# Attention outputs written from PSUM into the operand of the gated MLP, weight rows loaded in the matching order, and one attention phase in every MLP step

## The chip, the cores and the metric

The kernel runs on one core of one Trainium2 chip. The metric is the device time of one execution in microseconds, as the median of several runs. Everything is float32 at the boundary. The large matrix products take their operands as two float32r parts, high and low.

## What is computed

```python
# attention: B, H, S, D = 4, 8, 768, 48
for t in range(S):
    cur = einsum('bhd,bhe->bhde', u * k[t], v[t])
    y[t] = einsum('bhd,bhde->bhe', r[t], state + cur)
    state = w[t][..., None] * state + einsum('bhd,bhe->bhde', k[t], v[t])
x = y.transpose(0, 2, 1, 3).reshape(3072, 384)      # channel = 48 * head + d
x = ((x @ w_a) * (x @ w_b)) @ w_out                 # 384 -> 1536 -> 384
h = x @ w_in                                        # 384 -> 2048
out = (maximum(h, 0) + alpha * minimum(h, 0)) @ w_out2
```

## The kernel before, in words

**Attention** (in `front`). The sequence recurrence is replaced by a tree. Inside blocks of 64 positions the weights of query and key pairs are built in a leaf step and in levels of 2 to 64, by multiplying decays into keys and queries; between blocks a state per head is carried. The work is cut into 8 duos. A duo is half the sequence (384 tokens) of four pairs of heads of one batch. It has two streams, j = 0 and 1, of two pairs each (a pair of one stream is a unit); the two heads of a pair lie in partitions 0 to 47 and 64 to 111. A duo has 11 phases: leaf products (phase 0), the products of w on DVE (phase 1, no TensorE work), five levels of 192 small products (2 to 6; levels 1 to 4 on blocks of 64, level 5 on 32), the turning of keys (7), key-value products of stream 0 and of stream 1 (8, 9), and outputs (10): `weighted_values` of both streams, then `state_products`, accumulated in banks 0 to 3 of the PSUM tensor `products`, with the heads of stream 1 crossed (partition 64 * (hd ^ j)).

**From attention to the MLP.** ACT copies the outputs to `f_y` (`copy_y`, L478), SP stores them to `y` in DRAM by four DMAs per duo (`store_y`, L306), then loads a tile of 384 tokens and all 384 channels into `x_in` (`load_tile`, L333; `load_x`, L114), ACT makes `x_hi` (L122) and DVE `x_lo` (L126). `f_y` also holds the products of w of a duo, so `products_of_w` (L754) waits until the stores have landed.

**The gated MLP** runs on 8 tiles of 384 tokens in 12 steps each (f, 128 hidden channels): `up_a` and `up_b` of 9 products of 128x384 each (3 channel blocks by 3 products hi*hi, lo*hi, hi*lo; L132), ACT's copy of a, DVE's product `g_sb` (L862), ACT's `g_hi`, DVE's `g_lo` (L868) and `down`, again 9 products. The tile's result goes to `x_in` (`copy_x2`, L507) and to DRAM for the second MLP, called leaky, which follows in a block of its own and is not touched but for the counts that it waits for.

**Order.** Every engine runs a list written out by hand. The first BEFORE_TILES = 13 phase steps run alone; then `step_at(g)` (L167) puts one phase into each of the steps f = 0 to 10 of every tile, none into f = 11. In a step with a phase the order on TensorE is up_a(g), down(g - 1), up_b(g), phase; the b product then shares bank 4 with a (`shared_bank`, L179, and `b_ps`, L271) and has to wait for ACT's copy of a. Elsewhere it goes to bank 0 or 1.

**Weights.** A piece is 128x768 numbers (256 columns of w_a or w_b, or 256 rows of w_out). SP loads it into one of three `stage` buffers with one DMA (L97), ACT makes the high part (L103), POOL the low part (L108). Piece n is loaded once piece n - 3 is split. The first EARLY = 5 pieces are split in the opening, in steps 6, 7, 8, 9 and 11; `new_pieces(f)` (L189) names those of tile 0's steps. The queue of SP is in order: per duo it issues v and r (phase 2), k (7), the stores of y, the loads of w (10), and between them pieces and x.

## Time and profile before

| | us |
|---|---|
| median of 3 runs | 1073.93 (1073.47 to 1075.55) |
| the profiled execution, its own time | 1074.55 |
| its span, first to last instruction | 1072.7 |
| TensorE (PE) busy | 1011.1, 94% |
| DVE busy | 502.3, 47% |
| ACT busy | 302.5, 28% |
| POOL busy | 218.8, 20% |
| mean granted TensorE clock | 0.98 |

PE is the row of TensorE's products, PEld that of its weight loads, SPq and ACTq the queues that issue DMAs. A row of a group gives the busy time, the mean time of one in ns, then the idle time of the engine just before them and what ended it. A row of the timeline gives start and length in us; what stands in brackets is the idle time before it and what ended it. The granted clock is a share of 2.4 GHz.

### The profile page before, as it was taken

How to read it: one execution, taken by the hardware profiler on the slowest of the kernel's cores; microseconds unless marked ns; L12 is line 12 of the kernel's file. 1: busy time of each engine (PE TensorE's matmuls, PEld its weight loads, DVE VectorE, ACT ScalarE, POOL GpSimd, SP SyncE). 2: the span in 40 equal slices, each digit the busy share in tenths (PEclk: the TensorE clock that was granted, in tenths of full speed). 3: DMA queues.
4: the chain of work that ended last, by engine and by line, in shares of the span. 5: the costliest groups of instructions: out<-in, count | busy, mean ns of one | idle time of the engine just before them, and what ended most of it. 6: DMA issues, size and time to landing. Idle time of an engine off the chain costs nothing. (4 is left out here: it accounts for less than half of the span.)

```text
span 1072.7 us, 28894 instructions
## 1 busy us (share of the span) xinstructions
PE 1011.1 (94%) x12448; PEld 982.5 (92%) x12448; DVE 502.3 (47%) x978; ACT 302.5 (28%) x612; POOL 218.8 (20%) x165
## 2 busy tenths in 40 slices
PE   4658899999999999999999998999999999999998
PEld 4548899899899999899999998999999999999998
DVE  6367344344353453443353223645454545454554
ACT  2423422422323323224213332421212121222221
POOL 3456424024043132131140140400000000000000
PEclk9769999999999999999999999999999999999999
DMA  6342450140231221311300221310101010101000
GB/s 175 101 135 76 116 156 3 45 125 6 65 101 28 72 72 28 92 51 28 94 24 3 73 98 60 96 45 1 45 2 45 1 44 0 44 0 46 1 23 23
DMA packets 45687, 60.09 MB, mean 56 GB/s; under 512 B 4096, under 2 KB 45568, under 8 KB 45568
## 3 DMA queue, kind: packets, MB, share of 16 engines
q1 hardware_dynamic: 44240, 58.21, 18.3%
q8 instruction: 94, 1.54, 0.6%
q10 hardware_dynamic: 1328, 0.13, 0.1%
q14 instruction: 25, 0.20, 0.1%
HBM read 44.17 MB, written 14.16 MB: 54 GB/s over the span
## 5 line engine op out<-in xcount | busy, mean ns | idle before, releaser
L134 PE MATMUL products<-x_hi,weights_hi 128*128 128x384 f32 x576 | 202.9, 352 | 22.7 <-DVE x_lo L128 21.0
L135 PE MATMUL products<-x_lo,weights_hi 128*128 128x384 f32 x576 | 195.8, 340 | 0.0
L136 PE MATMUL products<-x_hi,weights_lo 128*128 128x384 f32 x576 | 195.6, 340 | 0.0
L862 DVE TENSOR_TENSOR g_sb<-a_g,products 128x384 f32<-128x384 f32 x96 | 53.2, 554 | 275.6 <-PE products L136 188.9
L995 DVE TENSOR_SCALAR leaky_low<-leaky_h_ps,leaky_al 128x384 f32<-128x384 f32 x128 | 79.0, 617 | 176.5 <-PE leaky_h_ps L136 176.4
L947 ACT ACTIVATE leaky_g_hi<-leaky_g_sb 128x384 fp32r<-128x384 f32 x128 | 67.3, 525 | 295.7 <-DVE leaky_g_sb L1000 295.7
L134 PEld LDWEIGHTS products<-x_hi,weights_hi 128*128 128x128 f32 x576 | 109.2, 190 | 28.9 <-DVE x_lo L128 23.1
L388 POOL TENSOR_TENSOR r_in<-r_in,f_y 112x384 f32<-112x384 f32 x80 | 104.9, 1325 | 143.9 <-PE products L602 143.9
L434 ACT ACTIVATE g_hi<-g_sb 128x384 fp32r<-128x384 f32 x96 | 50.4, 525 | 250.4 <-DVE g_sb L862 250.4
L136 PEld LDWEIGHTS products<-x_hi,weights_lo 128*128 128x128 f32 x576 | 109.5, 190 | 0.0
L135 PEld LDWEIGHTS products<-x_lo,weights_hi 128*128 128x128 f32 x576 | 109.4, 190 | 0.0
L134 PE MATMUL acc<-g_hi,weights_hi 128*128 128x384 f32 x288 | 98.6, 343 | 3.6 <-DVE g_lo L868 3.6
L136 PE MATMUL acc<-g_hi,weights_lo 128*128 128x384 f32 x288 | 98.1, 341 | 0.0
L135 PE MATMUL acc<-g_lo,weights_hi 128*128 128x384 f32 x288 | 97.6, 339 | 0.0
L434 ACT ACTIVATE a_g<-products 128x384 f32<-128x384 f32 x96 | 47.1, 491 | 135.4 <-PE products L136 135.3
L868 DVE TENSOR_TENSOR g_lo<-g_sb,g_hi 128x384 fp32r<-128x384 f32 x96 | 61.7, 643 | 40.7 <-ACT g_hi L434 40.6
L977 DVE TENSOR_TENSOR leaky_g_lo<-leaky_g_sb,leaky_g_hi 128x384 fp32r<-128x384 f32 x128 | 74.7, 584 | 5.3 <-ACT leaky_g_hi L947 4.7
L602 PEld LDWEIGHTS products<-r_in,k_in 48*64 48x64 f32 (+1 forms) x3840 | 61.5, 139 | 16.4 <-issue 11.4
L602 PE MATMUL products<-r_in,k_in 48*64 48x32 f32 (+1 forms) x3840 | 66.4, 223 | 6.5 <-DVE a_sb L784 3.8
L1000 DVE SCALAR_TENSOR_TENSOR leaky_g_sb<-leaky_h_ps,leaky_low 128x384 f32<-128x384 f32 x128 | 70.5, 551 | 0.3
L134 PE MATMUL leaky_h_ps<-x_hi,ahead_hi 128*128 128x384 f32 x192 | 65.4, 341 | 2.4 <-PEq L197 2.4
L134 PE MATMUL leaky_acc<-ahead_hi,leaky_g_hi 128*128 128x384 f32 x192 | 64.6, 337 | 0.7 <-DVE leaky_g_lo L977 0.7
(72 smaller groups left out, 1844.3 us busy)
## 6 DMA issues: line engine op xcount, KB each, us to landing
x_in<-y_dram SPq DMA_DIRECT2D x16, 576.0 KB, 4.6
k_in<-in_k_dram SPq DMA_DIRECT2D x16, 336.0 KB, 4.2
r_in<-in_r_dram SPq DMA_DIRECT2D x16, 336.0 KB, 5.2
w_v<-in_w_dram SPq DMA_DIRECT2D x16, 336.0 KB, 5.0
stage<-in_w_out_dram SPq DMA_DIRECT2D x14, 384.0 KB, 3.1
w_v<-in_v_dram SPq DMA_DIRECT2D x16, 288.0 KB, 3.1
y_dram<-f_y SPq DMA_DIRECT2D x32, 144.0 KB, 2.7
y_dram<-x_in SPq DMA_DIRECT2D x8, 576.0 KB, 3.3
```

Source lines behind the costliest of these rows:

```text
L134: pe.matmul(out, w_hi, x_hi, start=first, stop=False)
L135: pe.matmul(out, w_hi, x_lo, start=False, stop=False)
L136: return pe.matmul(out, w_lo, x_hi, start=False, stop=last)
L388: pool.tensor_tensor(halves(t, h, 1), halves(t, h, 1), decay(j, h, 0), ALU.mult).then_inc(r_stepped[j], 1)
L434: return act.activation(out, in_, ACT.Copy)
L602: last = pe.matmul(view(products, level_bank(phase, hd) + 32 * (CH * j + c), [[1, 32]], rows, BLOCK * par), key_blocks(k_in[j], hd, c, par ...
L862: dve.tensor_tensor(g_sb[:, :], a_g[:, :], b_ps(g), ALU.mult).then_inc(g_ready, 1)
L868: dve.tensor_tensor(g_lo[f % 2][:, :], g_sb[:, :], g_hi[f % 2][:, :].bitcast(F32), ALU.subtract).then_inc(g_lo_ready, 1)
L947: return act.activation(out_, in_, ACT.Copy)
L977: return dve.tensor_tensor(out_, in_, hi.bitcast(F32), ALU.subtract)
L995: dve.tensor_scalar(low[f % 2][:, :], h, 0.0, al[:, f:f + 1], ALU.min, ALU.mult).then_inc(low_ready, 1)
L1000: dve.scalar_tensor_tensor(g_sb[f % 2][:, :], h, 0.0, low[f % 2][:, :], ALU.max, ALU.add).then_inc(g_ready, 1)
```

## The change

- `copy_outputs` (ACT) and `lower_outputs` (DVE) read the output banks of `products` and write the high and the low part of x: stream 0's two units and stream 1's first unit (rows 0 to 111) go to the three channel blocks of `x_parts`, which is `x_hi` and `x_lo` in one tensor. Stream 1's second unit goes to the second half of `f_y`, and six DMAs of 16 rows move it to rows 48 to 63 and 112 to 127 of the three blocks (`move_rows`; for duo 0 two of them on ACT's queue). The DRAM trip of y, `store_y`, `load_tile` and the x splits of the first MLP go, except those of x for the second MLP's first tile.
- The channels of x now lie in another order, so the rows of w_a and w_b are loaded in that order: six DMAs per piece (`heads_in_place`) of 48 rows x 2 KB, 48 rows x 1 KB and 16 rows x 3 KB, twice. The number of bytes is the same.
- BEFORE_TILES is 11, and every step from g = 0 has a phase until all are done (g = 76). Step 0 counts as a shared-bank step. EARLY is 3: three pieces are split in the opening, their high parts in phases 2 to 4, their low parts in phases 7 to 9; the others in tile 0.
- `weighted_values` of stream 0 runs in phase 9, after the key-value products of stream 1.
- In the opening, DVE merges stream 0's leaf before it steps stream 1's keys, and stream 1's leaf before the five smaller products of w of stream 1. For duo 0 the preparation of duo 1's keys and of its second stream's queries stands behind the outputs.

```diff
 PIECE = 2 * P * KT
-EARLY = 5
+EARLY = 3
 AHEAD = 8
...
 F_AT = {2: 0, 4: S // 2, 8: S // 2 + S // 4, 16: S - S // 8, 32: S - S // 16, 64: S - S // 32}
-BEFORE_TILES = PHASES + 2
-EARLY_AT = [6, 7, 8, 9, 11]
-X_SPLIT = 10
+BEFORE_TILES = PHASES
+LO_AT = [7, 8, 9]
+HI_AT = [2, 3, 4]
+X_LOAD, X_SPLIT = 4, 8
+OUTPUTS, MOVES = 6, 6
 STAGES = 3
...
         self.x_in = sb("x_in", [P, KT * TT])
-        self.x_hi = [sb(f"x_hi{j}", [P, KT * TT], F32R) for j in range(2)]
-        self.x_lo = [sb(f"x_lo{j}", [P, KT * TT], F32R) for j in range(2)]
+        self.x_parts = [sb(f"x_parts{j}", [P, 2 * KT * TT], F32R) for j in range(2)]
+        self.x_hi, self.x_lo = ([x[:, part * KT * TT:(part + 1) * KT * TT] for x in self.x_parts] for part in range(2))
         self.staged, self.x_loaded = [sem(f"staged{j}") for j in range(STAGES)], sem("x_loaded")
...
-        self.pieces, self.number, self.place = [], {}, {}
+        self.pieces, self.number, self.place, self.staged_by = [], {}, {}, {}
         for ups, down in up_down:
...
                 for name, w in ups:
-                    self._add(name, n, w[:, 2 * P * n:2 * P * (n + 1)].rearrange("(k p) n -> p k n", p=P), [[2 * P, KT], [1, 2 * P]])
-                self._add("down of " + ups[0][0], n, down[2 * P * n:2 * P * (n + 1), :].rearrange("(f p) m -> p f m", p=P), [[DM, 2], [1, DM]])
-
-    def _add(self, name, n, source, dims):
-        self.number[name, n] = len(self.pieces)
-        self.pieces.append((source, dims))
+                    columns = w[:, 2 * P * n:2 * P * (n + 1)]
+                    if len(ups) > 1:
+                        self._add(name, n, self.heads_in_place(columns))
+                    else:
+                        self._add(name, n, [(0, P, 0, [[2 * P, KT], [1, 2 * P]], columns.rearrange("(k p) n -> p k n", p=P))])
+                self._add("down of " + ups[0][0], n, [(0, P, 0, [[DM, 2], [1, DM]],
+                                                       down[2 * P * n:2 * P * (n + 1), :].rearrange("(f p) m -> p f m", p=P))])
+    def heads_in_place(self, columns):
+        dims = [[1, 2 * P]]
+        parts = []
+        for block in range(2):
+            row0, last = 64 * block, D * (7 - block)
+            parts.append((row0, D, 0, [[2 * P, 2]] + dims, columns[0:2 * E2, :].rearrange("(k r) n -> r k n", k=2)[D * block:D * (block + 1)]))
+            parts.append((row0, D, 4 * P, dims, columns[D * (5 - block):D * (6 - block), :]))
+            parts.append((row0 + D, 16, 0, [[2 * P, KT]] + dims, columns[last:last + D, :].rearrange("(k p) n -> p k n", p=16)))
+        return parts
+    def _add(self, name, n, parts):
+        at = self.number[name, n] = len(self.pieces)
+        self.pieces.append(parts)
+        self.staged_by[at] = self.staged_by.get(at - STAGES, 0) + 16 * len(parts)
...
     def load_piece(self, sp, n):
-        source, dims = self.pieces[n]
         if n >= STAGES:
             sp.wait_ge(self.w_ready, n - STAGES + 1)
-        sp.dma_start(view(self.stage[n % STAGES], 0, dims, P), source).then_inc(self.staged[n % STAGES], 16)
+        for row0, rows, at, dims, source in self.pieces[n]:
+            sp.dma_start(view(self.stage[n % STAGES], at, dims, rows, row0), source).then_inc(self.staged[n % STAGES], 16)
...
         (hi, _), at = self.place[n]
-        act.wait_ge(self.staged[n % STAGES], 16 * (n // STAGES + 1))
+        act.wait_ge(self.staged[n % STAGES], self.staged_by[n])
         act.activation(hi[:, at:at + PIECE], self.stage[n % STAGES][:, :], ACT.Copy).then_inc(self.w_hi_ready, 1)
...
-    tile, f = divmod(g, F1)
-    step = BEFORE_TILES + PHASES * tile + f
-    return step if f < PHASES and step < DUOS * PHASES else None
+    step = BEFORE_TILES + g
+    return step if step < DUOS * PHASES else None
...
-    return slot_at(g - 1) and slot_at(g)
+    return g == 0 or (slot_at(g - 1) and slot_at(g))
...
                 return BANK * (2 * j + side)
+            def output_parts(n):
+                hi, lo = shared.x_hi[n % 2], shared.x_lo[n % 2]
+                last_hi, last_lo = f_y[:, S:S + TT].bitcast(F32R), f_y[:, S + TT:2 * S].bitcast(F32R)
+                units_of_0 = (0, 2, hi[0:ROWS, 0:2 * TT], lo[0:ROWS, 0:2 * TT])
+                units_of_1 = ((1, 1, last_hi, last_lo), (0, 1, hi[0:ROWS, 2 * TT:3 * TT], lo[0:ROWS, 2 * TT:3 * TT]))
+                parts = []
+                for j, par, group in ((1, 0, units_of_1), (1, 1, units_of_1), (0, 0, (units_of_0,)), (0, 1, (units_of_0,))):
+                    for unit, units, hi_ap, lo_ap in group:
+                        ps = view(products, stream_bank(j, par) + TT // 2 * unit, [[BLOCK, HALF * units], [1, BLOCK]])
+                        tokens = [ap.rearrange("p (c t) -> p c t", t=P)[:, :, BLOCK * par:BLOCK * (par + 1)] for ap in (hi_ap, lo_ap)]
+                        parts.append((j, ps, *tokens))
+                return parts
+            def move_rows(engine, n, q, row0):
+                to = shared.x_parts[n % 2][row0 + D:row0 + 64, :].rearrange("p (h c) -> p h c", h=2)[:, :, q * TT:(q + 1) * TT].bitcast(F32)
+                engine.dma_start(to, f_y[row0 + 16 * q:row0 + 16 * q + 16, S:2 * S].rearrange("p (h t) -> p h t", h=2)).then_inc(moved, 16)
...
-                def store_y(n, j):
-                    first = 4 * (n // 2) + 2 * j
-                    sp.wait_ge(copied, copies(n, "outputs", j, 1))
-                    for hd in range(2):
-                        sp.dma_start(y[first:first + 2, hd, :, TT * (n % 2):TT * (n % 2 + 1)].rearrange("u d s -> d u s"),
-                                     view(f_y, S * j, [[TT, 2], [1, TT]], D, 64 * (hd ^ j))).then_inc(y_stored[j], 16)
+                def move_last_unit(n):
+                    sp.wait_ge(copied, outputs_copied(n, OUTPUTS - 1))
+                    sp.wait_ge(lowered, outputs_lowered(n, OUTPUTS - 1))
+                    for q in range(KT if n > 0 else 2):
+                        for row0 in (0, 64):
+                            move_rows(sp, n, q, row0)
...
                     elif phase == 10:
-                        store_y(n, 0)
-                        store_y(n, 1)
-                        if n == 0:
-                            load_tile(0)
+                        move_last_unit(n)
                         if n + 1 < DUOS:
...
                             load_w(n + 1, 1)
-
-                def load_tile(tile):
-                    b, half = divmod(tile, 2)
-                    if tile > 0:
-                        sp.wait_ge(shared.x_ready, tile)
-                    if tile > 1:
-                        sp.wait_ge(shared.x2_stored, 16 * (tile - 1))
-                    if tile < TILES:
-                        for j in range(2):
-                            sp.wait_ge(y_stored[j], 32 * (tile + 1))
-                    shared.load_x(sp, b % B, half)
...
                         shared.store_x2(sp, *divmod(tile - 1, 2))
-                    if f == X_SPLIT - 2:
-                        load_tile(tile + 1)
+                    if tile == TILES - 1 and f == X_LOAD:
+                        sp.wait_ge(shared.x2_stored, 16 * tile)
+                        shared.load_x(sp, 0, 0)
                 sp.wait_ge(x2_copied, TILES)
                 shared.store_x2(sp, B - 1, 1)
-                for j in range(2):
-                    sp.wait_ge(y_stored[j], 32 * DUOS)
+                sp.wait_ge(moved, 16 * MOVES * DUOS)
...
-                def copy_y(n, j):
-                    act.wait_ge(products_done[j], after(n, 9))
-                    for par in range(2):
-                        copy(view(f_y, S * j + BLOCK * par, [[P, CH], [1, BLOCK]]),
-                             view(products, stream_bank(j, par), [[BLOCK, CH], [1, BLOCK]])).then_inc(copied, 1)
+                def copy_outputs(n):
+                    if n >= 2:
+                        act.wait_ge(b_done, F1 * (n - 1))
+                    for j, ps, hi, _ in output_parts(n):
+                        act.wait_ge(products_done[j], after(n, 9))
+                        copy(hi, ps).then_inc(copied, 1)
...
                     elif phase == 10:
-                        copy_y(n, 0)
-                        copy_y(n, 1)
+                        copy_outputs(n)
+                        if n == 0:
+                            act.wait_ge(lowered, OUTPUTS)
+                            for row0 in (0, 64):
+                                move_rows(act, n, 2, row0)
...
                         prepare_r(n + 1, 0)
-                    elif phase == 8 and n + 1 < DUOS:
+                    elif phase == (10 if n == 0 else 8) and n + 1 < DUOS:
                         prepare_k(n + 1, 0)
                         prepare_r(n + 1, 1)
-                    elif phase == 9 and n + 1 < DUOS:
+                    if phase == (10 if n == 0 else 9) and n + 1 < DUOS:
                         prepare_k(n + 1, 1)
...
                     act.wait_ge(down_done, F1 * (tile + 1))
-                    act.wait_ge(shared.x_ready, tile + 2)
+                    act.wait_ge(shared.x2_stored, 16 * tile)
+                    if tile == TILES - 1:
+                        act.wait_ge(shared.x_ready, 1)
                     for m in range(KT):
...
                     attend_late(step)
-                    if step in EARLY_AT:
-                        shared.split_hi(act, EARLY_AT.index(step))
-                    if step == PHASES:
-                        shared.split_x_hi(act, 0, 0)
+                    if step in HI_AT:
+                        shared.split_hi(act, HI_AT.index(step))
                 for g in range(TILES * F1):
...
                     for j in range(2):
-                        weighted_values(n, j)
-                    for j in range(2):
                         pe.wait_ge(r_stepped[j], 6 * n + 6)
...
                         turn_keys(n, 1)
-                    elif 8 <= phase <= 9:
-                        key_values(n, phase - 8)
+                    elif phase == 8:
+                        key_values(n, 0)
+                    elif phase == 9:
+                        key_values(n, 1)
+                        weighted_values(n, 0)
                     elif phase == 10:
+                        weighted_values(n, 1)
                         outputs(n)
...
                     if f == 0:
-                        pe.wait_ge(shared.x_ready, tile + 1)
+                        pe.wait_ge(copied, outputs_copied(tile, OUTPUTS - 1))
+                        pe.wait_ge(lowered, outputs_lowered(tile, OUTPUTS - 1))
+                        pe.wait_ge(moved, 16 * MOVES * (tile + 1))
                     if tile == 0 and f % 2 == 0:
...
                         pe.wait_ge(g_ready, from0(g - 1))
-                    if f >= 10 and tile < 6:
-                        pe.wait_ge(merged, merges(tile + 2, 0, f - 10))
-                    elif f == 9 and tile == 6:
-                        pe.wait_ge(copied, copies(DUOS - 1, "outputs", 0, 1))
+                    if step_at(g) is None:
+                        pe.wait_ge(copied, outputs_copied(DUOS - 1, OUTPUTS - 1))
+                        pe.wait_ge(lowered, outputs_lowered(DUOS - 1, OUTPUTS - 1))
+                    elif not shared_bank(g):
+                        pe.wait_ge(merged, merges(step_at(g) // PHASES, 0, g % 2))
                     up(g, "w_b", b_ps(g), b_done)
...
             def _(dve):
-                def products_of_w(n, first, streams):
+                def products_of_w(n, first, streams, parts=(True, True)):
...
                     for j in range(first, first + streams):
-                        dve.wait_ge(y_stored[j], 32 * n)
+                        dve.wait_ge(moved, 16 * MOVES * n)
                         dve.wait_ge(w_loaded[j], 16 * (n + 1))
-                    dve.tensor_tensor(of(f_y, 0, 1, S // 2), of(w_v, 0, 2, S // 2), of(w_v, 1, 2, S // 2), ALU.mult).then_inc(f_done, 1)
+                    if parts[0]:
+                        dve.tensor_tensor(of(f_y, 0, 1, S // 2), of(w_v, 0, 2, S // 2), of(w_v, 1, 2, S // 2), ALU.mult).then_inc(f_done, 1)
+                    if not parts[1]:
+                        return
                     for i, h in enumerate((4, 8, 16, 32, 64)):
...
+                def lower_outputs(n):
+                    if n >= 2:
+                        dve.wait_ge(b_done, F1 * (n - 1))
+                    for part, (j, ps, hi, lo) in enumerate(output_parts(n)):
+                        dve.wait_ge(copied, outputs_copied(n, part | 1 if part < 4 else part))
+                        dve.tensor_tensor(lo, ps, hi.bitcast(F32), ALU.subtract).then_inc(lowered, 1)
                 def attend_early(step):
...
                     n, phase = divmod(step, PHASES)
-                    if phase == 0:
+                    if phase == 0 and n > 0:
                         for j in range(2):
...
                         carry_states(n, phase - 8)
+                    elif phase == 10:
+                        lower_outputs(n)
...
                 dve.memset(products[:, :], 0.0).then_inc(products_cleared, 1)
-                for j in range(2):
-                    first_step_k(0, j)
-                    products_of_w(0, j, 1)
+                first_step_k(0, 0)
+                products_of_w(0, 0, 1)
                 dve.wait_ge(leaf_mask_loaded, 32)
                 dve.wait_ge(cleared, 1)
+                merge_leaf(0, 0)
+                first_step_k(0, 1)
+                products_of_w(0, 1, 1, (True, False))
+                merge_leaf(0, 1)
+                products_of_w(0, 1, 1, (False, True))
                 for step in range(BEFORE_TILES):
-                    if step == BEFORE_TILES - 1:
-                        shared.split_x_lo(dve, 0, 0)
                     attend_early(step)
```

## Rows read from the trace of the kernel before

**Rows 1.** The page: busy TensorE, and the costliest group of DVE in the MLP.

```profile
PE 1011.1 (94%) x12448; PEld 982.5 (92%) x12448; DVE 502.3 (47%) x978; ACT 302.5 (28%) x612; POOL 218.8 (20%) x165
...
L862 DVE TENSOR_TENSOR g_sb<-a_g,products 128x384 f32<-128x384 f32 x96 | 53.2, 554 | 275.6 <-PE products L136 188.9
```

**Rows 2.** Waits of TensorE, whole span: for what, us in total, times, longest.

```profile
PE products L134 <- DVE x_lo L128: 21.0, 7, 14.3
...
PE products L657 <- issue: 5.3, 4, 1.7
...
PE acc L134 <- DVE g_lo L868: 3.6, 4, 1.5
```

**Rows 3.** Timeline from the first outputs to the first MLP product.

```profile
42.14 2.59 PE L657 MATMUL products<-r_in,state 48*48 48x64 f32 x80
...
47.65 1.59 ACT L434 ACTIVATE f_y<-products 112x384 f32<-112x384 f32 x4
...
48.55 2.84 PE L579 MATMUL products<-r_leaf,k_scratch 48*64 48x64 f32 x96 [3.82 <-ACT f_y L434]
...
50.07 2.54 SPq L310 DMA_DIRECT2D y_dram<-f_y  x4
...
61.08 4.55 DVE L128 TENSOR_TENSOR x_lo<-x_in,x_hi 128x1152 fp32r<-128x1152 f32 x1 [8.58 <-ACT x_hi L124]
...
65.69 0.69 PE L134 MATMUL products<-x_hi,weights_hi 128*128 128x384 f32 x1 [14.30 <-DVE x_lo L128]
```

**Rows 4.** Windows: us, busy us and count of each engine, granted clock, DMA share, GB/s.

```profile
40.30:65.60 25.30, 6.75 (x224) 6.38 (x224) 6.99 (x9) 8.40 (x17) 8.20 (x6) 0.50 0.43 129
65.70:71.00 5.30, 5.30 (x17) 5.30 (x18) 4.84 (x6) 1.96 (x3) 3.45 (x2) 0.50 0.09 24
```

**Rows 5.** Timeline of the opening, around the first merges of the leaf.

```profile
10.98 0.56 DVE L823 TENSOR_TENSOR k_in<-k_in,w_v 112x384 f32<-112x384 f32 x1 [0.89 <-DMA w_v<-in_w_dram]
...
13.03 1.32 DVE L766 TENSOR_TENSOR f_y<-f_y 112x192 f32<-112x192 f32 x5
...
14.28 1.98 DVE L784 COPY_PREDICATED a_sb<-leaf_mask,products 128x384 f32<-128x384 int32 x4
...
16.31 2.79 PE L602 MATMUL products<-r_in,k_in 48*64 48x32 f32 x96 [3.84 <-DVE a_sb L784]
```

**Rows 6.** Timeline of a duo in the middle, from its last output products.

```profile
287.42 0.64 PE L657 MATMUL products<-r_in,state 48*48 48x64 f32 x26 [1.19 <-issue]
...
291.36 1.44 SPq L282 DMA_DIRECT2D w_v<-in_w_dram  x2
...
296.05 1.19 POOL L394 TENSOR_TENSOR k_in<-k_in,w_v 112x384 f32<-112x384 f32 x1 [31.98 <-DMA w_v<-in_w_dram]
...
301.20 0.95 DVE L762 TENSOR_TENSOR f_y<-w_v 112x768 f32<-112x768 f32 x1
...
302.19 1.71 DVE L766 TENSOR_TENSOR f_y<-f_y 112x384 f32<-112x384 f32 x5
```

**Rows 7.** The stores of y: issue time in ns, and time to landing.

```profile
L310 SPq DMA_DIRECT2D y_dram<-f_y x32: 327/440/1052, 50.1 to 590.5; - x32
...
DMA to landing us min/median/max: 2.2/2.7/4.0
```

**Rows 8.** Timeline of POOL in the first step of tile 0.

```profile
72.55 2.87 POOL L388 TENSOR_TENSOR r_in<-r_in,f_y 112x384 f32<-112x384 f32 x2 [3.39 <-PE products L602]
75.37 3.95 POOL L111 TENSOR_TENSOR weights_lo<-stage,weights_hi 128x768 fp32r<-128x768 f32 x2
```

**Rows 9.** Groups by line: ACT's high parts of the first MLP's weights.

```profile
L106 ACT ACTIVATE weights_hi<-stage 128x768 fp32r<-128x768 f32 x18 | 14.9, 838 | 1.3 <-DMA stage<-in_w_a_dram 1.2
```

**Rows 10.** Timeline of TensorE: duo 1's last output products.

```profile
133.11 0.33 PE L657 MATMUL products<-r_in,state 48*48 48x64 f32 x8 [1.71 <-issue]
```

**Rows 11.** DMA queues from 130 to 134 us: packets, MB, share of 16 engines.

```profile
q8 instruction: 1, 0.02, 1.4%
```

**Rows 12.** Window of one duo's period, from duo 2's outputs to duo 3's.

```profile
288.00:362.60 74.60, 73.36 (x1270) 70.01 (x1268) 32.42 (x73) 23.63 (x52) 20.12 (x16) 1.00 0.21 62
```

42 lines of the change are left out of this document (23 added, 19 removed).

## The prediction

> **What bounds the kernel now.** I read the page first. TensorE is busy 1011.1 us, 94% of the span [rows 1]. So a change pays where it fills TensorE's idle time, and nowhere else. The waits of TensorE say what that time is: 21.0 us for the DVE that makes x_lo (7 times, the longest 14.3), 5.3 us of "issue" ahead of the output products of line 657, 3.6 us for g_lo [rows 2]. The other waits lie in the opening attention phases. Next I read the opening in order of time [rows 3]. The first duo's output products end at 44.7. ACT copies them to f_y only at 47.65 (it is preparing the next duo's keys), the leaf of duo 1 runs at 48.55, the stores to DRAM are issued from 50.07, x_in is loaded behind them, x_lo takes 4.55 us from 61.08 beside a busy POOL, and the first MLP product starts at 65.69. From 40.3 to 71.0 the granted clock is 0.5, the lower level, 1.2 GHz [rows 4]. TensorE had just become mostly idle before it fell, and it rose 5.3 us after dense work began again.
>
> **The change, part by part.** Times are on the span of the profiled execution. T is the end of a duo's output products.
>
> 1. *First leaf merges moved.* DVE now merges stream 0 in the idle 0.89 us it has before the second stream's w, and leaves the five small f_y products (1.32 us) behind the second merge [rows 5]. The merges were four in 1.98 us; two go ahead (0.99, of which about 0.1 sticks out), and 1.32 moves behind. TensorE's level 1 starts at about 14.2, not 16.3, and everything up to the outputs moves by 2.1 us. DVE has 1.3 us to spare during level 1, so the postponed products cost nothing. Outputs end at 44.7 - 2.1 = 42.6. Moving ACT's weight splits to phases 2 to 4, where it idles, adds nothing.
>
> 2. *Outputs straight to x, first tile.* For duo 0 the key preparations now stand behind the copies, so ACT starts at 42.7. Four copies of 384 columns took 1.59 us [rows 3]; six copies, four of half width, I take at 2.3 (between 1.6 and 2.6). DVE subtracts behind them; the last, like the product of a step at 0.55 us [rows 1], ends at 45.6. Then rows move by DMA: four issues on SP, two on ACT. The nearest row is the store of f_y: issue 0.33 to 1.05 us, median 0.44; landing 2.2 to 4.0 us, median 2.7 [rows 7]. The last of four issues starts 1.6 to 2.4 us after the first (I take 2.0), and I take 2.7 for the landing: 50.4. The first up product starts there instead of at 65.69: -15.3. Two things come back. The leaf of duo 1, done in the old idle time, now runs inside the MLP at full clock: 2.84 us at half clock [rows 3] gives about +1.6. And step 0 now uses the shared bank, so the b product waits for ACT's copy of a: +0.8 (a copy of about 0.4 and two handovers; 0.5 to 1.2). The half-clock tail of 5.3 us stays. Part sum **-12.9** (-14.5 to -9).
>
> 3. *x for later tiles.* Besides the 14.3 there are six x_lo waits of 21.0 - 14.3 = 6.7 us at tile starts [rows 2]. They go with x_lo itself: **-6.7**. Late next is the move. Duo 1's outputs end at step 10 and tile 1 starts at step 12, with 27 MLP products and the leaf between. One duo's period is 74.6 us for 12 steps and 11 phases [rows 12], 6.2 us per step, and 6.4 with this leaf. The path is copies and subtraction 3.0, six issues 2.6 to 3.3, landing 2.7: T + 8.7 against T + 6.4. **+2.3** (0 to +5). For duo 2 the slack is one step more, then two, and so on: nothing. A stall can also drop the clock for a short stretch, as after the opening [rows 4]: I add **+1.0** (0 to +3).
>
> 4. *Weight rows loaded to fit.* A w_a or w_b piece is now six DMAs instead of one. This is the part whose price I know least. It matters in tile 0, where five pairs of such pieces are split (EARLY goes from 5 to 3) and four of them loaded. A piece three ahead is loaded only when POOL has split the old one. The loop of a pair is: POOL's two splits, 3.95 us [rows 8]; twelve issues at 0.44, 5.3; the last landing, 2.7; ACT's split of 0.84 [rows 9]. Sum 12.8 us, while two steps give 12.4. POOL also has its 2.87 us of query steps per phase ahead of the splits [rows 8], but two steps hold both. So the loop is just on the path: 0.4 us in each of four pairs, plus some collisions of ACT's waiting split with g_hi. **+2.5**. Below, tile 0's g_lo waits of 3.6 us vanish; above, issues at 1.05 give rival A. One rule speaks against this part. The Trainium skill, "DMA: Bandwidth & Descriptors", "Rules for kernel authors", wants many small transfers made into one, since below 64 KB one pays mostly overhead; half of the parts and all the moved rows are of 48 KB. The stores here, 144 KB each, lie closer to one whole piece than to such a part, so no row contradicts it. If by that rule every part cost as much as the slowest store's issue, the time would be rival A's.
>
> 5. *A phase per step, no step left out.* The moves stand in SP's queue ahead of the loads of w. Today w is issued 3.3 us after T and POOL starts 4.7 us after that issue [rows 6]. Now the issue comes at T + 3.0 + 3.0 = T + 6.0 to 6.7, POOL starts at T + 11.4, and its four operations of 1.2 us end at T + 16.1. Level 1 was two full steps and an empty one behind the leaf; now it comes at T + 16.3. It just fits. DVE's products of w (0.95 and 1.71 us alone [rows 6], up to twice that beside POOL) now sit directly ahead of the step whose g_lo TensorE needs at T + 19.8; I get T + 19.4 to 20.0. **+1.5** over six duos (0 to +12).
>
> 6. *Weighted values of stream 0 in phase 9.* In the output burst the wait of 1.71 us comes in the middle of line 657's products, while one packet moves on the instruction queue [rows 10, 11]: the burst of 190 products with their weight loads outruns the fetching of code. 48 of them (0.7 us) leave the burst for a phase that had half a load. 5.3 us of such waits [rows 2] become perhaps half: **-2.6** (-5.3 to 0).
>
> 7. *Rest.* ACT and DVE lose eight x splits and gain copies of similar length. DRAM traffic falls, on no path. The second MLP is untouched.
>
> Sum: -12.9 - 6.7 + 2.3 + 1.0 + 2.5 + 1.5 - 2.6 = **-14.9 us**. The profiled execution took 1074.55 us around its span of 1072.7, and gives 1059.65; the median of the runs is 0.6 lower, so 1059.0.
>
> **The rivals.** *A, slower: SP becomes the bound.* Place: the six-part weight loads of tile 0 and the six moves ahead of each w. If an issue costs 0.9 to 1.05 us, which the slowest stores show [rows 7], not 0.44, the loop of a pair grows by 12 x 0.5 = 6 us, four times: +24. Level 1 of six duos also waits some 2 us. Time 1080 or more. It decides from about 0.7 us per issue on, where the gain is gone. Against it: the median is 0.44 and the traffic is light. Chance 0.08. *B, the DRAM trip was only part of the wait.* If the rows land as late as the slowest stores and x is ready near 54, if ACT's and DVE's queues hold the copies, and the crowding of part 5 costs 1 us a duo, the saving shrinks to some 7 us: 1067. Chance 0.18, and 0.02 more that nothing is left of it (1072 to 1076). *C, all stalls go.* Code fetching never lags and tile 0 flows freely: 1051. Chance 0.12. *Forecast*: 1059, chance 0.60.
>
> **The numbers.** About 0.2% is what a measurement of this kernel can tell from no change, 2 us. Rival A is slower; the 0.02 counts as the same; the rest, 0.90, is faster. The range 1051 to 1071 takes in the forecast with its bounds, B and most of C; it leaves out A and the lower tail.
>
> **What would show it.** Right: first up product near 50 with no load from y before it; x_lo gone from TensorE's waits; one wait of 2 to 3 us at the start of tile 1 for a DMA; "issue" ahead of line 657's successor halved; few waits for w pieces in tile 0. Wrong: SP's issues of weight parts end to end through tile 0 with ACT waiting on stage; TensorE waiting for r_in or k_in at every level 1; a start of the MLP later than 54.

## The result, and the profile after

The changed kernel takes 1067.47 us, the median of 5 runs (1065.47 to 1069.02), against 1074.19 us for the kernel before in the same comparison: ratio 0.9932 with an interval of 0.9914 to 0.9949. That is 6.7 us faster. The forecast was 14.9 us faster. The time lies inside the range of the prediction, but less than half of the saving that it forecast came.

The profiled execution took 1068.26 us, with a span of 1066.5. TensorE's row of the page answers to [rows 1]:

```profile
PE 1013.6 (95%) x12448; PEld 984.7 (92%) x12448; DVE 521.1 (49%) x1018; ACT 293.7 (28%) x620; POOL 217.7 (20%) x165
```

**Where the time went.** The first up product starts at 52.86 instead of 65.69 [rows 3], 12.8 us earlier. From there to the end the kernel before needed 1007.0 us and this one 1013.6. So 6.6 us are given back inside the MLP tiles. The prediction had 15.3 and +0.4 for these two stretches: it was 2.5 short in the first, 6.2 in the second. Two windows from just behind the first product, first of the kernel before, then of the one after, split the second. The columns are the window, its length, and the busy time of PE, PEld, DVE, ACT and POOL, then the granted clock, the DMA share and GB/s.

```profile
66.00:1072.00 1006.00, 981.18 (x11408) 954.74 (x11407) 469.25 (x915) 281.73 (x568) 190.82 (x139) 0.99 0.17 51
```

```profile
53.00:1066.00 1013.00, 985.56 (x11504) 958.79 (x11504) 493.20 (x954) 275.18 (x577) 196.16 (x143) 0.99 0.16 45
```

TensorE is busy 4.4 us longer (the 96 products of duo 1's leaf are among it now) and idle 27.4 us instead of 24.8. The idle time hardly moves although x_lo's waits are gone, so new waits took their place. TensorE's waits in the kernel after (waited for, us in total, times, longest) name them; these answer to [rows 2]:

```profile
PE acc L153 <- DVE g_lo L927: 13.1, 8, 3.8
PE products L618 <- ACT r_leaf L473: 10.6, 2, 7.7
PE products L153 <- issue: 10.5, 2, 7.6
PE acc L153 <- ACT x_in L468: 2.6, 1, 2.6
...
PE products L641 <- POOL r_in L422: 1.1, 1, 1.1
...
PE products L153 <- ACT a_g L468: 0.6, 1, 0.6
```

x_lo is gone, and the 5.3 us of "issue" in the output burst too. "issue" ahead of L153 is the wait for the moved rows: 7.63 us in the opening and 2.85 at tile 1. New are 13.1 us for g_lo, against 3.6 before, and 2.6 and 1.1 us for ACT and POOL. Looked up one by one in the timeline, they fall into two sets. Three lie in tile 0: 3.82 us up to 91.73, 0.88 and 1.85. Six lie some 20 us behind the outputs of a duo, at five places for duos 2 to 6: 2.65, 1.11 with 1.49 behind it, 1.48, 1.78 and 1.54, together 10.05 us. Each set had one experiment or more.

The second set, in the duo that answers to [rows 6]: SP's queue, DVE, POOL and TensorE of the kernel after, from the timeline (start, length; in brackets the idle time before).

```profile
285.06 3.77 SPq L316 DMA_DIRECT2D x_parts<-f_y  x6
288.88 2.32 SPq L329 DMA_DIRECT2D w_v<-in_w_dram  x2
...
294.15 1.21 POOL L428 TENSOR_TENSOR k_in<-k_in,w_v 112x384 f32<-112x384 f32 x1 [34.52 <-DMA w_v<-in_w_dram]
295.31 1.52 POOL L422 TENSOR_TENSOR r_in<-r_in,w_v 112x384 f32<-112x384 f32 x1
296.78 1.91 POOL L428 TENSOR_TENSOR k_in<-k_in,w_v 112x384 f32<-112x384 f32 x1
298.65 1.47 POOL L422 TENSOR_TENSOR r_in<-r_in,w_v 112x384 f32<-112x384 f32 x1
...
295.69 1.95 DVE L807 TENSOR_TENSOR f_y<-w_v 112x768 f32<-112x768 f32 x1
297.68 4.91 DVE L813 TENSOR_TENSOR f_y<-f_y 112x384 f32<-112x384 f32 x5
302.58 0.56 DVE L921 TENSOR_TENSOR g_sb<-a_g,products 128x384 f32<-128x384 f32 x1
...
300.18 0.90 PE L641 MATMUL products<-r_in,k_in 48*64 48x32 f32 x48 [1.11 <-POOL r_in L422]
304.34 0.44 PE L153 MATMUL acc<-g_hi,weights_hi 128*128 128x384 f32 x1 [1.49 <-DVE g_lo L927]
```

The duo's outputs end at 282.1. The six moves wait for the copies and take 3.77 us of the queue, and w is issued at T + 6.8, just past the upper end that the prediction gave (T is the end of a duo's output products, here 282.1). POOL starts 5.3 us later, T + 12.0 here, and then its four operations lie over all six of DVE's products of w. These take 1.95 and 4.91 us instead of 0.95 and 1.71 [rows 6]. g_sb stands behind them on DVE, so it, g_hi and g_lo come late, and TensorE waits.

### The profile page after: what moved, and what is told of

Its sections match the earlier page's. It is cut to its first block and busy times, and to the rows that moved or that the text cites. A ratio compares the mean times of both kernels' runs of the same rounds, so it can differ in the third digit from the quotient of the medians.

```text
span 1066.5 us, 29038 instructions
## 1 busy us (share of the span) xinstructions
PE 1013.6 (95%) x12448; PEld 984.7 (92%) x12448; DVE 521.1 (49%) x1018; ACT 293.7 (28%) x620; POOL 217.7 (20%) x165
## 3 DMA queue, kind: packets, MB, share of 16 engines
q8 instruction: 94, 1.54, 0.6%
## 5 line engine op out<-in xcount | busy, mean ns | idle before, releaser
L153 PE MATMUL products<-x_parts,weights_hi 128*128 128x384 f32 x576 | 204.0, 354 | 11.9 <-issue 10.5
L154 PE MATMUL products<-x_parts,weights_hi 128*128 128x384 f32 x576 | 196.9, 342 | 0.0
L155 PE MATMUL products<-x_parts,weights_lo 128*128 128x384 f32 x576 | 196.4, 341 | 0.0
L153 PEld LDWEIGHTS products<-x_parts,weights_hi 128*128 128x128 f32 x576 | 110.3, 192 | 16.7 <-issue 12.3
L422 POOL TENSOR_TENSOR r_in<-r_in,f_y 112x384 f32<-112x384 f32 x80 | 99.8, 1261 | 112.1 <-PE products L641 109.3
L153 PE MATMUL acc<-g_hi,weights_hi 128*128 128x384 f32 x288 | 99.6, 346 | 15.7 <-DVE g_lo L927 13.1
L154 PEld LDWEIGHTS products<-x_parts,weights_hi 128*128 128x128 f32 x576 | 110.4, 192 | 0.0
L155 PEld LDWEIGHTS products<-x_parts,weights_lo 128*128 128x128 f32 x576 | 110.4, 192 | 0.0
L927 DVE TENSOR_TENSOR g_lo<-g_sb,g_hi 128x384 fp32r<-128x384 f32 x96 | 67.3, 701 | 43.1 <-ACT g_hi L468 42.5
L153 PEld LDWEIGHTS acc<-g_hi,weights_hi 128*128 128x128 f32 x288 | 55.0, 191 | 18.7 <-DVE g_lo L927 18.6
L153 PE MATMUL leaky_h_ps<-x_parts,ahead_hi 128*128 128x384 f32 x192 | 64.7, 337 | 2.4 <-PEq L225 2.4
```

The lines of the kernel that those rows point to most:

```text
L153: pe.matmul(out, w_hi, x_hi, start=first, stop=False)
L154: pe.matmul(out, w_hi, x_lo, start=False, stop=False)
L155: return pe.matmul(out, w_lo, x_hi, start=False, stop=last)
L422: pool.tensor_tensor(halves(t, h, 1), halves(t, h, 1), decay(j, h, 0), ALU.mult).then_inc(r_stepped[j], 1)
L927: dve.tensor_tensor(g_lo[f % 2][:, :], g_sb[:, :], g_hi[f % 2][:, :].bitcast(F32), ALU.subtract).then_inc(g_lo_ready, 1)
```

## The experiments

Each edit is against the changed kernel unless another is named. Each ratio is to the kernel before, measured beside it; differences of ratios are turned into time with 1074 us. By the intervals of the two ratios such a difference is good to some 3 us either way.

**1. w ahead of the moves.** Only the order in SP's queue changes.

```diff
                     elif phase == 10:
-                        move_last_unit(n)
                         if n + 1 < DUOS:
                             load_w(n + 1, 0)
                             load_w(n + 1, 1)
+                        move_last_unit(n)
```

> The changed kernel with the loads of the next duo's w issued ahead of the six moves of rows. Theory X (w comes late behind the moves, so POOL's first steps of keys and queries collide with DVE's products of w, and DVE is late with g_sb of the phase-2 step): POOL starts about 6 us after a duo's outputs, not 9; DVE's products of w take 0.95 + 1.7 us again, not 1.95 + 4 to 5; the phase-2 waits of TensorE of 1.1 to 2.7 us (10 us over five duos, and one clock dip of 1.5) vanish; tile 1's wait for the moves grows by about 1.1 us. Time 1057 to 1060 us. Rival Y (the products of w directly ahead of a step with a phase are too much for DVE, whenever w comes): the waits stay at 1 us or more per duo, time 1066 to 1069 us.

Measured: 1052.35 us (1047.87 to 1053.06), ratio 0.9800 (0.9783 to 0.9817). These two lines are worth 14.2 us by the ratios (0.9932 less 0.9800), more than the 8 to 10 us that were expected. The same duo in its timeline:

```profile
270.50 0.81 SPq L329 DMA_DIRECT2D w_v<-in_w_dram  x2
...
273.43 3.79 SPq L316 DMA_DIRECT2D x_parts<-f_y  x6
...
274.58 1.18 POOL L428 TENSOR_TENSOR k_in<-k_in,w_v 112x384 f32<-112x384 f32 x1 [26.45 <-DMA w_v<-in_w_dram]
...
283.62 0.95 DVE L807 TENSOR_TENSOR f_y<-w_v 112x768 f32<-112x768 f32 x1
284.61 1.70 DVE L813 TENSOR_TENSOR f_y<-f_y 112x384 f32<-112x384 f32 x5
```

w is issued the moment the outputs end, POOL is through by 279.6, and DVE's products of w stand alone at 0.95 and 1.70 us. Of TensorE's waits between 145 and 636 us one is left:

```profile
PE acc L153 <- DVE g_lo L927: 0.3, 1, 0.3
```

The moves still begin where they did, behind the copies: w's two issues fit into the time in which ACT and DVE copy. Tile 1 waited 2.66 us for its rows, not more than 2.85. So the order in the changed kernel bought nothing that this run shows.

**2. Half of the moves ahead of w.**

```diff
-                    for q in range(KT if n > 0 else 2):
-                        for row0 in (0, 64):
-                            move_rows(sp, n, q, row0)
+                    rows = [(q, row0) for q in range(KT if n > 0 else 2) for row0 in (0, 64)]
+                    for at, (q, row0) in enumerate(rows):
+                        if at == len(rows) // 2 and n + 1 < DUOS:
+                            load_w(n + 1, 0)
+                            load_w(n + 1, 1)
+                        move_rows(sp, n, q, row0)
...
                         move_last_unit(n)
-                        if n + 1 < DUOS:
-                            load_w(n + 1, 0)
-                            load_w(n + 1, 1)
```

> The changed kernel with the loads of w issued behind three of the six moves. A smaller dose of the same cause. Theory X (what counts is whether POOL's four steps are done before DVE's products of w start, 13.1 us after the outputs): w is issued at +4.9 and lands at +8.9, POOL runs from +9 to +13.6, DVE's products take about 3 us, TensorE's phase-2 waits stay under 0.5 us; tile 1 waits about 4 us for the last moves, 1.1 more than in the change. Time 1053 to 1056 us. Rival (every place behind a move costs its share, 2 us of time per move): half of the 14 us come back, 1059 to 1061 us.

Measured: 1054.95 us, ratio 0.9834 (0.9814 to 0.9853). The waits behind the outputs are gone here too, with w three issues (1.8 us) earlier than after. So the cost is not so much per move: it sets in somewhere between three and six moves ahead of w. The same duo shows why. POOL ends at 290.25, 0.3 us before DVE's products of w start:

```profile
289.06 1.19 POOL L422 TENSOR_TENSOR r_in<-r_in,w_v 112x384 f32<-112x384 f32 x1
290.59 0.95 DVE L807 TENSOR_TENSOR f_y<-w_v 112x768 f32<-112x768 f32 x1
```

What w takes from the later moves now shows: tile 1 waits 4.56 us and the opening 10.03.

**3. Weight pieces whole.** w_a and w_b are loaded by one DMA per piece again; the placing of the weight rows is left out.

```diff
-                    if len(ups) > 1:
+                    if len(ups) > 9:
                         self._add(name, n, self.heads_in_place(columns))
```

> The changed kernel with w_a and w_b pieces loaded by one DMA each, in plain row order, so the rows do not match x: this leaves out the placing of weight rows, all else is as in the change. Theory P (the six-part loads cost the opening about 2 us, because the second stream's w lands 2 us later, and make tile 0's waits for g_lo of 6.6 us and two clock dips of 1.5): the first up product starts near 50.5, not 52.9, and tile 0 loses at most 3 us in waits. Time 1059 to 1061 us. Rival (tile 0's waits are POOL's splits locking out DVE, as before, whatever the loads): only the opening's 2 us come back, 1065 to 1066 us.

Measured: 1061.79 us, ratio 0.9883 (0.9860 to 0.9905), 5.3 us less than the changed kernel, with 3.1 us either way. The first up product starts at 51.0; with six parts it starts between 49.9 and 52.9 in the runs that leave the moves alone, so the opening gives nothing that shows. Tile 0, from its first up product to tile 1's, takes 85.3 us instead of 91.1. Together with experiment 1:

> The loads of w first, and w_a and w_b pieces by one DMA each in plain row order (leaves out the placing of weight rows). Theory P (six parts per piece cost tile 0 about 5 us: ACT's high part waits for the last part, holds up g_hi and pushes g_lo into POOL's splits): the wait of 3.8 us at the end of step 4 goes, tile 0 and its clock dips give back 4 to 6 us, 1047 to 1048.5 us. Rival (what was won with whole pieces before was luck of the DMAs in the opening): 1051 to 1053 us, and the waits for g_lo in tile 0 stay at 6 us.

Measured: 1045.08 us, ratio 0.9731 (0.9715 to 0.9746). The two gains add: 14.2 and 5.3 make 19.5, and 21.6 came, again more than was expected. But what do the six parts cost: issue time, or the moment at which the last of them lands?

**4. ACT's high parts behind g_hi.** In tile 0 ACT waits for a piece before it makes g_hi of the step. Here it makes g_hi first. w is ahead of the moves as in experiment 1, the parts stay six.

```diff
+                    act.wait_ge(g_ready, g + 1)
+                    act.wait_ge(down_done, from0(g - 1))
+                    copy(g_hi[f % 2][:, :], g_sb[:, :]).then_inc(g_hi_ready, 1)
                     if tile == 0:
                         for piece in new_pieces(f):
                             shared.split_hi(act, piece)
-                    act.wait_ge(g_ready, g + 1)
-                    act.wait_ge(down_done, from0(g - 1))
-                    copy(g_hi[f % 2][:, :], g_sb[:, :]).then_inc(g_hi_ready, 1)
```

> The loads of w first, and in tile 0 ACT makes the high parts of weights behind g_hi, not ahead of it. Theory H (the long g_lo wait is g_hi standing behind a split that waits for its last part): the waits for g_lo in tile 0 fall from 6.4 us to under 3, time 1047.5 to 1050 us. Rival L (the loop of load, high part, low part then turns too slowly): TensorE waits for weight pieces (lines of the first products of even steps, for POOL or DMA) by more than what g_lo gives back, 1052 us or more.

Measured: 1044.28 us (1040.65 to 1045.64), ratio 0.9715 (0.9694 to 0.9735). That is 9.1 us less than experiment 1, where 2.3 to 4.8 were expected, and at least as much as whole pieces gave there (7.4; the intervals overlap). The timeline shows why. First the kernel after, in the middle of tile 0: ACT, DVE, POOL, TensorE.

```profile
85.80 0.85 ACT L125 ACTIVATE weights_hi<-stage 128x768 fp32r<-128x768 f32 x1 [2.98 <-DMA stage<-in_w_b_dram]
86.55 0.51 ACT L468 ACTIVATE g_hi<-g_sb 128x384 fp32r<-128x384 f32 x1
...
84.70 0.56 DVE L921 TENSOR_TENSOR g_sb<-a_g,products 128x384 f32<-128x384 f32 x1 [1.71 <-issue]
...
87.10 4.58 DVE L927 TENSOR_TENSOR g_lo<-g_sb,g_hi 128x384 fp32r<-128x384 f32 x1 [0.94 <-ACT g_hi L468]
...
85.64 2.10 POOL L422 TENSOR_TENSOR r_in<-r_in,f_y 112x384 f32<-112x384 f32 x2 [1.44 <-PE products L641]
87.70 3.56 POOL L130 TENSOR_TENSOR weights_lo<-stage,weights_hi 128x768 fp32r<-128x768 f32 x2
...
91.73 0.60 PE L153 MATMUL acc<-g_hi,weights_hi 128*128 128x384 f32 x1 [3.82 <-DVE g_lo L927]
```

And the same place with g_hi first:

```profile
84.01 0.52 ACT L468 ACTIVATE g_hi<-g_sb 128x384 fp32r<-128x384 f32 x1 [3.31 <-DVE g_sb L921]
84.44 1.57 ACT L125 ACTIVATE weights_hi<-stage 128x768 fp32r<-128x768 f32 x2
...
84.80 0.55 DVE L927 TENSOR_TENSOR g_lo<-g_sb,g_hi 128x384 fp32r<-128x384 f32 x1
...
85.76 5.19 DVE L825 TENSOR_TENSOR k_in<-k_in,f_y 112x384 f32<-112x384 f32 x1
...
86.91 3.62 POOL L130 TENSOR_TENSOR weights_lo<-stage,weights_hi 128x768 fp32r<-128x768 f32 x2
```

In the kernel after g_sb is done at 85.26, but ACT stands for 2.98 us at the last part of w_b and comes to g_hi at 86.55. g_lo then starts 0.6 us before the end of a query step of POOL, behind which its two low parts follow at once, and takes 4.58 us instead of 0.55. With g_hi first, g_lo is done before POOL starts. The long operation is now a step of the keys, 5.19 us, and TensorE waits only 0.47 us for it. Tile 0 takes 82.8 us and waits 0.7 for g_lo.

**5. The same edit without experiment 1's.**

> The changed kernel with ACT's high parts behind g_hi in tile 0, and nothing else. Theory: this cost sits in tile 0 alone and the late w in the later tiles alone, so they add: 8 us off 1067.5, 1058 to 1061 us; tile 0's waits for g_lo under 1.5 us, the phase-2 waits of 1.1 to 2.7 us all still there. Rival (they share time, the one hides the other): less than 5 us off.

Measured: 1058.25 us, ratio 0.9868 (0.9840 to 0.9897): 6.9 us less than the changed kernel, tile 0 at 82.1 us, the waits behind the outputs still there (2.65, 2.01, 1.78, 1.49, 1.86). The two faults are separate.

**6. g_hi first, w first and whole pieces** (the placing of the weight rows is left out).

> The loads of w first, the high parts behind g_hi, and whole pieces in plain row order (leaves out the placing of weight rows). Theory (the six parts cost time only because ACT waits for the last part ahead of g_hi): once that wait is behind g_hi the parts are nearly free, within 1.5 us of the 1044.3 with six parts. Rival (the parts cost SP and POOL time of their own): another 4 us or more come off, 1040 us or less.

Measured: 1043.72 us, ratio 0.9727 (0.9699 to 0.9755), against 0.9715 with six parts. Once ACT no longer stands in front of g_hi, six parts cost nothing that these runs can tell (whole pieces came out 1.3 us slower, with 3.7 either way). The Trainium skill, "DMA: Bandwidth & Descriptors", "Rules for kernel authors", would have small transfers made into one; here the measurement shows no gain from it once TensorE's next step does not stand behind the last part. ACT still waits 3.4 us for parts in experiment 4 and 1.6 us for whole pieces here, and it costs no time that shows.

**7. Weighted values back in phase 10.**

```diff
                         key_values(n, 1)
+                    elif phase == 10:
                         weighted_values(n, 0)
-                    elif phase == 10:
                         weighted_values(n, 1)
```

> The changed kernel with the weighted values of stream 0 back in phase 10. Theory F (the output burst outruns the fetching of code): waits marked issue of 1 to 1.7 us return inside the output products in three or four duos, +4 to +6 us less what they hide of other waits: 1070 to 1073 us. Rival (the waits went for another reason, such as the new alignment or the DRAM traffic that is gone): no such waits, within 1 us of 1067.5.

Measured: 1069.51 us (10 runs), ratio 0.9957 (0.9941 to 0.9972), 2.7 us more than the changed kernel, with 2.5 either way; 4 to 6 were expected. In TensorE's waits "issue" returns twice in the output products, 1.8 us in all, and once, 0.7 us, in front of an up product:

```profile
PE products L696 <- issue: 1.8, 2, 1.1
```

The place is the one that was named, but only two duos have such a wait, where three or four were expected, and only 1.8 of the 5.3 us of the kernel before come back. So the move explains a third of what vanished. Why the rest is gone is not shown.

**8. The first pieces of weights loaded later.** In the profiled execution after, w of the second stream landed just ahead of 12.97 us, when DVE takes it up, where the kernel before had 10.98 [rows 5]. The suspicion was the traffic of three pieces that are now loaded in eighteen parts.

```diff
-                for piece in range(STAGES):
-                    shared.load_piece(sp, piece)
                 for step in range(BEFORE_TILES):
                     attend(step)
+                    if step == 2:
+                        for piece in range(STAGES):
+                            shared.load_piece(sp, piece)
```

> The changed kernel with the first three weight pieces (13 DMAs) issued after the values and the next queries, not ahead of them. Theory P: the second stream's w lands near 11.0 us, not 13.0; level 1 starts near 14.2, not 16.0; everything after is 1.8 us earlier: 1065 to 1066 us. Rival (the opening waits for something else than the small parts, such as the first descriptors being slow): w lands at 12.5 or later and the time stays within 0.5 us of 1067.5.

Measured: 1066.38 us, ratio 0.9917 (0.9892 to 0.9941), not told from the changed kernel. w landed at 10.8 us, but with an unchanged opening it landed at 10.6 in experiment 7 and at 11.5 in experiment 1. The landing varies from run to run by 2 us, so the late landing needs no cause in the change. The time alone, 1.6 us less with 3.2 either way, could not have told. The suspicion isn't borne out.

**9. Only DVE's new opening order, put into the kernel before.**

```diff
-                for j in range(2):
-                    first_step_k(0, j)
-                    products_of_w(0, j, 1)
+                first_step_k(0, 0)
+                products_of_w(0, 0, 1)
...
+                merge_leaf(0, 0)
+                first_step_k(0, 1)
+                products_of_w(0, 1, 1, (True, False))
+                merge_leaf(0, 1)
+                products_of_w(0, 1, 1, (False, True))
```

> The kernel before with the change's order of DVE in the opening and nothing else of it. The forecast gave this part 2.1 us: level 1 starts near 14.2, not 16.3, the outputs of duo 0 end near 42.6, not 44.7, and the time is 2 us shorter, 1072 to 1073 us. Rival (the landing of the second stream's w, which has come between 10.6 and 12.9 us in the runs so far, sets the start of level 1): level 1 starts about 3.1 us after that landing, the gain is between 0.5 and 2.1 us, hard to tell from none.

Measured: 1071.88 us (12 runs) against 1073.41, ratio 0.9986 (0.9966 to 1.0006), not told from none, nor from the forecast 2.1 us. Level 1 starts at 14.67, 1.6 us earlier, and the first MLP product at 60.4, 5.3 earlier. Then this stands in the timeline of DVE and of TensorE:

```profile
66.10 7.44 DVE L769 TENSOR_TENSOR f_y<-f_y 112x96 f32<-112x96 f32 x3
...
75.29 0.69 PE L134 MATMUL acc<-g_hi,weights_hi 128*128 128x384 f32 x1 [6.72 <-DVE g_lo L875]
```

Three small products take 7.44 us beside POOL's query steps and low parts and hold g_sb behind them. The lead is lost within one tile: tile 1 starts at 151.64, against 151.15 in the kernel before. So in this execution a first product that came 5.3 us earlier was worth nothing; a gain in the opening counts only if tile 0 can keep it.

**10. Tile 1's moves on two queues.** Experiment 1, with two of duo 1's six moves on ACT's queue.

```diff
-                    for q in range(KT if n > 0 else 2):
+                    for q in range(KT if n > 1 else 2):
...
+                    if phase == 10 and n == 1:
+                        act.wait_ge(lowered, outputs_lowered(n, OUTPUTS - 1))
+                        for row0 in (0, 64):
+                            move_rows(act, n, 2, row0)
```

> The loads of w first, and for duo 1 two of the six moves on ACT's queue, behind its copy of a of the next step. Theory M (tile 1's wait of 2.7 us is the issue time of six moves, 0.63 us each, and one landing of 2.2): the wait falls by 1.2 us to about 1.4 and may take the clock dip behind it with it, 1049 to 1051 us. Rival (ACT then is late with g_hi or the copy of a in step 11, or the wait is not the issue time): same time within 0.7 us of 1052.3, and a new wait on ACT in steps 11 or 12.

Measured: 1050.29 us, ratio 0.9769 (0.9751 to 0.9787). The wait at tile 1 is 2.43 us, not the 1.4 that was expected. Each of the six moves lands on 16 DMA engines; 95 of these 96 landings came by 139.63 and one at 141.19, 1.6 us behind the others. In these microseconds one packet of code moves on the instruction queue (DMA queues from 138 to 142 us: packets, MB, share):

```profile
q1 hardware_dynamic: 115, 0.11, 14.4%
q8 instruction: 1, 0.02, 2.4%
```

It started at 138.6 and took 1.52 us. That it holds the last landing up is likely, but no run took it away. Without the late landing the wait would have been near 0.9 us (an estimate from these landings), so the split of the issues did what it should and one late landing hid it. The time lies in the forecast, although the wait that was to give it fell by only 0.2 us against experiment 1: in that it is luck. With g_hi first as well:

> The loads of w first, ACT's high parts behind g_hi in tile 0, and two of duo 1's moves on ACT's queue: a candidate for the best. If the splitting of the moves over two queues is worth its 1.2 us of issue time, 1042 to 1043.5 us; if the last landing is set by something else, such as a packet of code on one DMA engine, the same as with the first two edits alone, 1043.5 to 1045 us, and the wait ahead of tile 1 stays at 2 us or more.

Measured: 1042.68 us (1040.92 to 1044.55), ratio 0.9721 (0.9693 to 0.9748), the lowest median, but not told from experiment 4. The time is that of the first forecast, the wait ahead of tile 1 (2.19 us) that of the second; again one landing came late, at 133.63, with the others by 132.31, and a packet of code moved from 131.3 to 132.5. Either beats both kernels, the one before by 2.8%.

## Why the prediction was wrong

The direction and most prices held; two couplings between engines were mis-sized. The step that failed is part 5: its +1.5 us for w behind the moves was 12 to 14. By its steps:

**Part 1 and 2, the opening: 12.8 instead of 15.3.** The row for the moves was well chosen. From the end of the outputs to the first product it took 7.63 us, and 7.8 was forecast (50.4 less 42.6). The outputs ended at 45.23, not at 42.6. This is part 1: w of the second stream came 2.0 us later in this execution, and level 1 started at 15.98, against the forecast 14.2 and 16.31 before. From DVE's step with this w to level 1 it took 3.0 us instead of 5.3, so the new order gave what was forecast and the late landing took it away. In the experiments level 1 started between 13.7 and 15.6. The leaf cost +2.2 (1.6 forecast), the shared bank's wait 0.58 (0.8). "The half-clock tail of 5.3 us stays" did not hold: it was 8.2 us long (see the last section).

**Part 3: held.** The six x_lo waits, 6.7 us, are gone. Tile 1 waits 2.85 us (2.3 forecast). Its clock cost more. The windows of the kernel after in which the granted clock fell to 0.5 (its column stands third from the end) are:

```profile
91.90:95.30 3.40, 3.40 (x11) 3.40 (x12) 1.20 (x3) 0.00 (x0) 0.00 (x0) 0.50 0.47 119
122.60:126.00 3.40, 3.40 (x12) 3.02 (x10) 0.26 (x2) 0.27 (x1) 1.83 (x1) 0.50 0.25 88
143.10:149.90 6.80, 5.99 (x19) 6.02 (x20) 0.07 (x1) 0.49 (x1) 4.00 (x4) 0.50 0.36 104
231.80:235.20 3.40, 3.40 (x13) 3.40 (x12) 0.77 (x1) 0.00 (x0) 0.00 (x0) 0.50 0.50 181
```

Each comes on a wait of TensorE just named. 3.4 us at half the clock do the work of 1.7, so tile 1's 6.8 cost up to 3.4, where +1.0 was put down. Against it stand three such stretches of the kernel before (at 81, 211 and 665 us) which vanished, up to 5.1 us that the prediction didn't count as a gain. No run shows why a given wait brings such a stretch or not.

**Part 4: the right place, the wrong mechanism.** The prediction counted the loop from load to split, found it "just on the path" and took +2.5. Experiment 3 says 5.3. The issues cost what was assumed: median 0.43 us. What failed is the half sentence "some collisions of ACT's waiting split with g_hi". That was the whole of it, and it is multiplied by POOL: 1.3 us lost at ACT push g_lo into POOL's low parts, and 3.8 us come out at TensorE. Two readings beside it were off as well: four of the six parts are of 48 KB, not half of them, and a store of 144 KB is nearer to a part of 96 KB than to a piece of 384, so the rows of the stores said less about parts than the prediction took from them. The measured 0.43 us now settles it.

**Part 5: the step that failed.** Forecast +1.5, with bounds of 0 and 12. The waits behind the outputs are 10.05 us, the stretch at half clock behind the first of them up to 1.7 more, 11.8; experiment 1 gives 14.2, with 2.6 either way. Every time up to POOL's start was forecast within 1 us (w at T + 6.0 to 6.7, POOL at T + 11.4). The error is in the sentence "It just fits". It laid POOL's four operations at 1.2 us each, as if nothing lengthened them, and DVE's products at up to twice their length. But the two lengthen each other. POOL's four took 5.9 us (294.15 to 300.1), DVE's six 6.9, where 2.66 was their time alone and 5.3 their double. g_lo, forecast for T + 19.4 to 20.0, was done at T + 22.2. Between that forecast and the T + 19.8 of TensorE's need lay a slack of -0.2 to 0.4 us, and it was treated as enough. "Up to twice" had no row, and one spoke against it: beside the same four operations of POOL x_lo took 4.55 us [rows 3], and alone, later in the kernel before, 1.35, a factor of 3.4:

```profile
303.81 1.35 DVE L128 TENSOR_TENSOR x_lo<-x_in,x_hi 128x1152 fp32r<-128x1152 f32 x1
```

Level 1 itself fitted, but for one wait of 1.11 us for POOL. The price of missing it was named only as the upper bound.

**Part 6: held in size, the mechanism only in part.** All 5.3 us of "issue" in the output burst are gone, not half. Experiment 7 puts the move at 2.7 us, with 2.5 either way; 2.6 was forecast. But only a third of the waits return with the move undone, so the other two thirds went for a reason that no run shows.

Added up behind the first product, these rows give: leaf and bank +2.8, x_lo -6.7, tile 1 +2.9, tile 0's g_lo +3.2 (6.55 less 3.3), duos 2 to 6 +10.1, issue and two small waits -6.5, clock +3.4, the opening's slow stretch (below), without the leaf, +0.5. That is +9.7, and +6.6 was measured; the 3 us between are not assigned.

**The rivals.** A, SP as the bound, didn't come: 0.43 us for a part and 0.59 for a move. B's number was met, by its last ground and not by its first: the rows did not land late, the crowding of part 5 did come, at 2.0 us for each of five duos instead of 1. Of C one half came, the waits of "issue" in the output burst went, and the other, a free tile 0, didn't. Its 1051 is close to what experiment 1 gives, but by an edit that C didn't have.

## What to carry to other kernels

When a load is moved behind other issues on its queue, follow it through to the last engine that uses it and ask which engine's work it will now overlap; a slack near zero that ends in an overlap of GpSimd and VectorE is a loss, not a fit. Put loads whose address and buffer are already free ahead of transfers that must wait for a computation: here two lines swapped were worth 14 us. And keep an engine's wait for slow data behind the short operation that the busiest engine needs next: a piece cut into six cost 5 us while ACT stood in front of g_hi, and nothing that the runs can tell once it stood behind.

## What the runs showed of the hardware that was not expected

**VectorE and GpSimd block each other, and one operation can be held through several.** The five small products of w took 1.70 us alone and 4.91 us beside POOL's steps; g_lo took 0.55 and 4.58, a step of keys 0.56 and 5.19 beside POOL's low parts. The long ones end just behind POOL's work (91.68 against 91.26, and 90.95 against 90.53). The Trainium skill, "SBUF — State Buffer", "SBUF: two separate sides", calls the port pair that the two share an exclusive lock, taken for a whole instruction, when VectorE's has two operands in SBUF and GpSimd's reads SBUF. The traces agree: g_sb, one of whose operands lies in PSUM, took 0.56 us at 116.81, in the middle of a low part of POOL (116.01 to 117.84), as it did alone. And they show more than that sentence: g_lo was held from 87.10 through the rest of one query step and through both low parts behind it, so the one that waits can lose its turn again.

**TensorE at half pace where the view shows a full clock.** In the opening of the kernel after, the view shows a granted clock of 1.00 through 48 to 60 us, and yet the first products follow each other by 0.32 us:

```profile
52.86 0.66 PE L153 MATMUL products<-x_parts,weights_hi 128*128 128x384 f32 x1 [7.63 <-issue]
53.32 0.52 PE L154 MATMUL products<-x_parts,weights_hi 128*128 128x384 f32 x1
53.64 0.52 PE L155 MATMUL products<-x_parts,weights_lo 128*128 128x384 f32 x1
```

From 62.2 us on it is 0.17. The kernel before had the pace of 0.32 up to 71 us with 0.50 in the record. The 1.00 is no measurement: the clock records of this trace begin at 61.1 us, those of the kernel before at 36.9, and where there is none the view shows 1.00. So in an opening the pace of equal products is the sign of the clock to go by. The slow stretch behind the first product is 8.2 us long (to 61.1), against 5.3 before.

**A short idle time can cost more than itself, and its length alone doesn't say whether.** In the kernel after, waits of TensorE of 3.8, 1.9, 2.9 and 2.7 us were each met by 3.4 or 6.8 us at a granted clock of 0.5; the waits of 1.5 to 1.8 us behind duos 4 to 6 were not, nor was one of 2.4 us at 659 us. In the kernel before, waits of 0.7, 1.4 and 2.4 us (up to 79.6, 209.8 and 663.8 us) were met, and those of 1.7 and 1.6 (up to 133.1 and 151.2) were not.
